# Delta attention, ELU network and top-2 experts on one core: narrower mask products, transpositions at the ends of periods, other gate chunks between the blocks

## Chip, core and metric

One core of one Trainium2 chip runs the whole program. The metric is its device time in microseconds, the median over runs.

## The reference, cut to what matters

```python
def _attn_ref(q, k, v, beta):                 # 4 x 8 heads, 768 positions, 48 wide
    k_n = k / (np.linalg.norm(k, axis=-1, keepdims=True) + 1e-06)
    state = zeros((B, H, D, D))
    for t in range(S):
        y[:, :, t] = q_t @ state
        v_old = k_t @ state
        state = state + beta_t * outer(k_t, v_t - v_old)

x = attention output as (3072, 384)
h = x @ w_in;  g = elu(h);  x = g @ w_out     # 384 -> 2048 -> 384
logits = x @ w_gate + log1p(exp(x @ w_noise)) * noise
the two best of 8 experts for each token:  relu(x @ w1[e]) @ w2[e], weighted and summed
```

The change touches the attention part and what is prepared beside it. Nothing in the ELU network or the experts is touched.

## The kernel before

The recurrence is done in chunks of 128 positions. A unit is one head of one chunk; 8 units (one batch entry, one chunk) are one n, and n runs from 0 to 23 (`NIT`). In each unit a 128 x 128 triangular system is solved in four steps of 32 rows (`BLK`), for which the four 32 x 32 diagonal blocks are inverted beforehand.

**Preparation.** TensorE computes the diagonal blocks in twelve groups, `diagonal_blocks(i)`, i from 0 to 11, called block 0 to block 11 here (64 matmuls each, which the profile shows as 128 with their weight loads). ScalarE copies each to SBUF (`take_blocks`). VectorE turns the blocks so that one lane holds one block (`to_set_lanes`), takes norms (`take_norms`) and runs the elimination column by column (`eliminate`, two operations a column, 31 columns). There are three groups of blocks. VectorE inverts the first one itself; it breaks off after `PREPARED` columns to turn and scale what the second group needs, and then ends its own 31 columns. GpSimd inverts groups 1 and 2: `POOL_COLUMNS` lists its columns, the first part (14 columns of group 1) after `scale_v(0)` and `scale_v(1)`, the others one part a period, each behind two `scale_v`, which wait for a chunk of v to be loaded. `place(g, s)` on VectorE turns a half of a finished group back; it waits for the last column of its group (`row_done`).

Between the blocks TensorE also does the gate: the product of w_out with the gate's weights, in 16 chunks. Chunk f is three transposes (`turn_output_weights`), a copy by ScalarE (`take_turned`) and three small matmuls (`gate_columns`), which come behind the transposes of chunk f + 1. `chunks_with(i)` says which chunks follow block i, on SyncE's queue, on TensorE and on ScalarE alike. When all 16 are turned, SyncE issues the loads of k for n = 0 to 3 and after them those of v for n = 2 and 3.

**Pairs.** After some filler matmuls (`keep_clock`), a loop over `PAIRS` = 12 periods m works on the two n = 2m and 2m + 1 (`solve`, `couple`, `outputs`, `updates`), and prepares the next two: `products_of_keys` on TensorE, `mask_products` on VectorE (which takes the products out of PSUM and zeroes what is not needed, writing `lq`; four pairs of operations in a period) and, from n = 4 on, `right_side`, which needs the v that GpSimd has scaled. The products have one PSUM buffer for each half, so the next products wait for the masks before. Each engine's order is written out by hand, in code order. A period is counted here from VectorE's first residual of it (`residuals(a, 1)`, L943).

From 275 us on the ELU network and the experts run.

Of the kernel before, what the change touches and what calls it, by code (L numbers as in the profile page):

```python
# [13 lines left out]
ALU = mybir.AluOpType  # L14
ACT = mybir.ActivationFunctionType
AX = mybir.AxisListType
P = 128
# [41 lines left out]
W_LOADED_WITH = {1: (2,), 2: (3,), 3: (4,), 4: (5,), 5: (0,), 6: (1,), 8: (6,), 9: (7, 8), 10: (9, 10, 11)}  # L59


PREPARED = 12
KEEP_BUSY = 29

# [3 lines left out]
def attention_outputs(nc, kv_dram, kqT_dram, beta_lanes, beta_turned, w_io, w_gn, masks, carried, inversion, w_parts,  # L70
# [13 lines left out]
    with ExitStack() as scope:  # L84
# [143 lines left out]

        def chunks_with(i):

            at = 2 * (i - KT_BUFS - 1)
            return (at, at + 1) if at >= 0 else ()

        def inverse_of(n, r):

# [23 lines left out]
        def _(sp):  # L259
# [81 lines left out]
            for i in range(KT_BUFS + 1, NIT // 2):  # L341
# [7 lines left out]
                    sp.dma_start(wgn, w_gn).then_inc(wgn_loaded, 16)  # L349
                for f in chunks_with(i):  # L350
                    load_output_weights(f)
            for f in chunks_with(NIT // 2):
                load_output_weights(f)
            sp.wait_ge(kqT_cleared, DEEP)
            for n in range(2, DEEP):
                load_kqT(n)
# [99 lines left out]
        def _(pe):  # L456
# [150 lines left out]
            for i in range(NIT // 2):  # L607
# [1 line left out]
                    products_of_keys(i // 2, i % 2)  # L609
                diagonal_blocks(i)  # L610
                gate_work(i)
            gate_work(NIT // 2)

            pe.wait_ge(blocks_taken, NIT // 2)
            gate_columns(FT1 - 1)
            pe.wait_ge(gate_taken, 1)
# [80 lines left out]
        def _(act):  # L697
# [78 lines left out]
            for i in range(NIT // 2):  # L776
# [4 lines left out]
                take_blocks(i)  # L781
                for f in chunks_with(i):
                    take_turned(f)
            for f in chunks_with(NIT // 2):
                take_turned(f)
            take_gate()
            act.wait_ge(cleared, len(by_pool))
            for n in range(2):
# [54 lines left out]
        def _(dve):  # L843
# [77 lines left out]
            def mask_products(n, c):  # L921
                dve.wait_ge(grams_done, 2 * n + c + 1)
                if n >= KEPT:

                    dve.wait_ge(y_done, n - KEPT + 1)
                for h in range(2):
                    to = lq[n % KEPT].rearrange("p (g a h) s t -> p g a h (s t)", g=2, h=2)[:, :, c * QP // 2:(c + 1) * QP // 2, h]
                    nc.vector.tensor_tensor(to, of_keys(h).rearrange("p g a s t -> p g a (s t)"),
                                            masks[:].rearrange("p g s t -> p g (s t)").unsqueeze(2).to_broadcast([P, 2, QP // 2, 2 * P]),
                                            ALU.mult).then_inc(masked, 1)  # L930

            def right_side(n):
                dve.wait_ge(ks_done[n % 2], (n - B) // 2 + 1)
# [51 lines left out]
            for m in range(PAIRS):  # L985
                a, b = 2 * m, 2 * m + 1
                past, more = m > 0, m < PAIRS - 1
                kept = past and b - 2 + B < NIT
                residuals(a, 1)
                if m == 1:  # L990
                    invert_root(2)
                if more:
                    mask_products(a + 2, 0)
                residuals(b, 1)
                if kept:
                    update_state(a - 2)
                if m == 1:
                    divide_by_root(2)
                if m == 3:
                    place(1, 0)  # L1000
                if m == 7:
                    place(2, 0)
                residuals(a, 2)
                if m == 1:
                    refine_root(2)
                if more:
                    mask_products(a + 2, 1)
                residuals(b, 2)
                if kept:
                    update_state(b - 2)  # L1010
                residuals(a, 3)
                if more and a + 2 >= B:
                    right_side(a + 2)
                if more:
                    mask_products(b + 2, 0)
                if more and b + 2 >= B:
                    right_side(b + 2)
                residuals(b, 3)
                if more:
                    mask_products(b + 2, 1)  # L1020
                if m == 0:
                    to_set_lanes(2, (5,))
                    square_norms(2)
                if m == 1:
                    gains(2)
                    turn_norms(2)
                if m == 4:
                    place(1, 1)
                if m == 7:
                    place(2, 1)  # L1030


TB = 384
# [955 lines left out]
```

## Time and profile before

| | |
|---|---|
| median of 3 runs | 1165.01 us (1163.78 to 1166.38) |
| the profiled execution | 1167.03 us |
| its span | 1165.3 us |
| preparation, until the first solve | 0 to 80 us |
| pairs | 80 to 275 us |
| ELU network and experts | 275 to 1165 us |
| TensorE busy over the span | 96% |
| TensorE clock granted, mean | 0.997 of full speed |

The span is the part of the execution that the profile records. Busy TensorE is not TensorE at its peak, since its matmuls are pipelined.

### The profile page before, as it was taken

What the parts mean: (1) busy time and instruction counts of PE and PEld (TensorE: products, weight loads), DVE (VectorE), ACT (ScalarE), POOL (GpSimd) and SP (SyncE); (2) the same over time, 40 slices, a digit from 0 to 9 for tenths busy, and PEclk for the clock granted to TensorE, in tenths of its full rate; (3) what the DMA queues carried; (4) which work ended last, traced back from release to release, by engine and by line L of the source; (5) the groups of instructions that cost most, each with busy time, mean ns of one, the idle gap of its engine ahead of it and who ended that gap; (6) DMA issues with size and microseconds to landing.
All of it is one profiled execution on the core that took longest, in us unless ns stands there. A gap on an engine that the chain in (4) does not pass through costs nothing.

```text
span 1165.3 us, 29047 instructions
## 1 busy us (share of the span) xinstructions
PE 1116.0 (96%) x11562; PEld 1069.2 (92%) x11562; DVE 647.7 (56%) x1552; ACT 462.6 (40%) x1048; POOL 355.7 (31%) x378
## 2 busy tenths in 40 slices
PE   4898999999999999999999999999999999999996
PEld 3786787888999999999999999999999999999995
DVE  4989787763465646565565657533434343434442
ACT  1236665884333343333333345323333333333331
POOL 5289995541002012020202102322223232322223
PEclk9999999999999999999999999999999999999998
DMA  7544657646996010010101011472424242434221
GB/s 158 126 128 105 166 135 172 164 139 237 366 360 208 25 58 35 27 41 20 41 20 42 22 43 66 172 235 73 170 79 166 86 157 94 147 103 140 61 69 53
DMA packets 82603, 137.30 MB, mean 118 GB/s; under 512 B 11050, under 2 KB 70034, under 8 KB 81466
## 3 DMA queue, kind: packets, MB, share of 16 engines
q1 hardware_dynamic: 68490, 87.97, 25.9%
q0 software_dynamic: 12992, 28.75, 7.7%
q10 hardware_dynamic: 1008, 18.97, 4.4%
q8 instruction: 83, 1.36, 0.5%
q14 instruction: 30, 0.25, 0.1%
HBM read 81.96 MB, written 53.77 MB: 116 GB/s over the span
## 4 chain that ended last, share of the span: by engine, by line
PE 74%; DVE 1%; issue 0%; ACT 0%; POOL 0%; ACTq 0%; POOLq 0%
PE ps_x L1426 18%; PE ps_x L1516 18%; PE ps_h L1415 18%; PE ps_h L1494 17%; PE ps_r L1474 2%; PE ps_r L1465 2%; DVE hg L1834 0%; ACT hg L1624 0%; POOL out_dram L1381 0%; DVE w_parts L1797 0%; PE ps_r L1533 0%; DVE x_raw L1827 0%; PE ps_r L1443 0%; ACT yT_d L1642 0%; PE ps_r L1441 0%
## 5 line engine op out<-in xcount | busy, mean ns | idle before, releaser
L1516 PE MATMUL ps_x<-hg,w_parts 128*128 128x400 f32 x1152 | 230.2, 346 | 0.0
L1426 PE MATMUL ps_x<-w_parts,hg 128*128 128x400 f32 x1152 | 229.7, 345 | 0.0
L1415 PE MATMUL ps_h<-xg,w_parts 128*128 128x384 f32 x1152 | 222.4, 338 | 0.0
L1494 PE MATMUL ps_h<-xg,w_parts 128*128 128x400 f32 x1116 | 220.6, 345 | 1.1 <-DVE w_parts L1797 1.1
L1426 PEld LDWEIGHTS ps_x<-w_parts,hg 128*128 128x128 f32 x1152 | 209.7, 188 | 0.0
L1834 DVE SCALAR_TENSOR_TENSOR hg<-ps_h,hg 128x400 fp32r<-128x400 f32 x128 | 73.6, 575 | 243.1 <-ACT hg L1624 242.6
L1415 PEld LDWEIGHTS ps_h<-xg,w_parts 128*128 128x128 f32 x1152 | 204.0, 188 | 2.5 <-DVE elu_parts L1691 2.5
L1494 PEld LDWEIGHTS ps_h<-xg,w_parts 128*128 128x128 f32 x1116 | 202.7, 188 | 4.0 <-issue 3.1
L1516 PEld LDWEIGHTS ps_x<-hg,w_parts 128*128 128x128 f32 x1152 | 206.1, 188 | 0.0
L1361 POOL DMA_INDIRECT xs_scratch<-x,rows_now x48 | 49.5, 1032 | 393.4 <-DVE rows_now L1771 294.7
L1624 ACT ACTIVATE hg<-ps_h 128x400 fp32r<-128x400 f32 x128 | 64.6, 505 | 256.5 <-PE ps_h L1494 256.5
L1573 ACT ACTIVATE hg<-elu_parts 128x384 fp32r<-128x384 f32 x128 | 67.2, 525 | 183.6 <-DVE elu_parts L1691 183.6
L1694 DVE TENSOR_TENSOR hg<-elu_parts,hg 128x384 fp32r<-128x384 f32 x128 | 71.6, 559 | 80.8 <-ACT hg L1573 80.8
L1381 POOL DMA_INDIRECT out_dram<-x_raw,token_now x48 | 48.6, 1012 | 175.7 <-DVE x_raw L1827 137.0
L1688 DVE TENSOR_SCALAR elu_parts<-expo 128x384 f32<-128x384 f32 x128 | 46.9, 366 | 85.0 <-ACT expo L1566 82.2
L1566 ACT ACTIVATE expo<-ps_h 128x384 f32<-128x384 f32 x128 | 62.1, 485 | 79.2 <-PE ps_h L1415 78.8
L1371 POOL DMA_INDIRECT x<-out_dram,token_now x45 | 47.4, 1052 | 127.0 <-DVE token_now L1816 115.9
L722 ACT ACTIVATE x_of<-psum 32x192 f32<-32x192 f32 x192 | 61.7, 321 | 59.8 <-PE psum L563 55.4
L1691 DVE SCALAR_TENSOR_TENSOR elu_parts<-ps_h,elu_parts 128x384 f32<-128x384 f32 x128 | 71.4, 558 | 4.4
L943 DVE TENSOR_TENSOR rhs<-rhs,psum 32x192 f32<-32x192 f32 x144 | 50.6, 351 | 31.7 <-PE psum L575 27.7
L253 POOL TENSOR_TENSOR inversion<-inversion 128x62 f32<-128x62 f32 (+15 forms) x62 | 55.5, 896 | 4.9
L526 PE MATMUL psum<-kqT 48*64 48x256 f32 (+1 forms) x768 | 45.3, 352 | 11.5 <-DMA kqT<-in_kqT_dram 7.4
(175 smaller groups left out, 1309.8 us busy)
## 6 DMA issues: line engine op xcount, KB each, us to landing
xs_scratch<-pads SPq DMA_DIRECT2D x2, 5502.0 KB, 41.9
x_rows<-xs_scratch SPq DMA_DIRECT2D x17, 614.1 KB
kqT<-in_kqT_dram SPq DMA_DIRECT2D x48, 192.0 KB, 4.0
carried<-in_w_dram ACTq DMA_DIRECT2D x3, 3072.0 KB, 11.2
w_raw<-in_w_dram ACTq DMA_DIRECT2D x3, 3072.0 KB, 11.4
xs_scratch<-pads SPq DMA_DIRECT2D x6, 1375.5 KB, 16.5
out_dram<-pads SPq DMA_DIRECT2D x1, 4800.0 KB, 30.1
xs_scratch<-pads SPq DMA_DIRECT2D x6, 786.0 KB, 9.0
```

Source lines behind the costliest of these rows:

```text
L253: vec.tensor_tensor(t, t, outer, ALU.subtract).then_inc(row_done[g], 1)
L722: nc.scalar.activation(x[n % KEPT][rows, half(g), :], ps_p[n % 2][rows, g * HALF_U * DH:(g + 1) * HALF_U * DH].rearrange("p (u d) -> p u d ...
L1415: mm = nc.tensor.matmul(ps_h[f % 2][:, 0:TB], wi[:, 1 - a, k, f * P:(f + 1) * P], xr[:, b, k, :], start=(i == 0), stop=(i == len(passes) - 1))
L1426: mm = nc.tensor.matmul(ps_x[t][:, 0:DG], act_r[:, f % RING, a, t * P:(t + 1) * P], wo[:, b, f, :], start=(f == 0 and i == 0), stop=(f == ...
L1494: mm = nc.tensor.matmul(ps_h[f % 2][:, 0:TR], w1, xg[:, b, k, :], start=(m == 0), stop=(m == len(passes) - 1))
L1516: mm = nc.tensor.matmul(ps_y[k][:, 0:TR], w2r[i][:, a, s, k * P:(k + 1) * P], hg[:, s % RING, b, :], start=(s == 0 and m == 0), stop=(s == ...
L1566: nc.scalar.activation(expo[:, f % 2], ps_h[f % 2][:, 0:TB], ACT.Exp).then_inc(exp_done, 1)
L1573: nc.scalar.activation(act_r[:, f % RING, 0], act_raw[:, f % 2], ACT.Copy).then_inc(act_hi, 1)
L1624: nc.scalar.activation(hg[:, f % RING, 0], ps_h[f % 2][:, 0:TR], ACT.Relu).then_inc(relu_hi, 1)
L1691: nc.vector.scalar_tensor_tensor(act_raw[:, f % 2], ps_h[f % 2][:, 0:TB], 0.0, expm[:, f % 2], ALU.max, ALU.add).then_inc(act_done, 1)
L1694: nc.vector.tensor_tensor(act_r[:, f % RING, 1], act_raw[:, f % 2], act_r[:, f % RING, 0], ALU.subtract).then_inc(act_split, 1)
L1834: nc.vector.scalar_tensor_tensor(hg[:, f % RING, 1], ps_h[f % 2][:, 0:TR], 0.0, hg[:, f % RING, 0], ALU.max, ALU.subtract).then_inc(relu_s ...
```

## The change

Five edits, and nothing else:

```diff
-PREPARED = 12
+PREPARED = 10
+GATE_WITH = {5: (0,), 6: (1,), 7: (2,), 8: (3, 4, 5), 9: (6, 7, 8), 10: (9, 10, 11), 11: (12, 13, 14, 15)}
...
         def chunks_with(i):
-            at = 2 * (i - KT_BUFS - 1)
-            return (at, at + 1) if at >= 0 else ()
+            return GATE_WITH.get(i, ())
...
-                    nc.vector.tensor_tensor(to, of_keys(h).rearrange("p g a s t -> p g a (s t)"),
-                                            masks[:].rearrange("p g s t -> p g (s t)").unsqueeze(2).to_broadcast([P, 2, QP // 2, 2 * P]),
-                                            ALU.mult).then_inc(masked, 1)
+                    nc.vector.tensor_tensor(to[..., BLK:], of_keys(h).rearrange("p g a s t -> p g a (s t)")[..., BLK:],
+                                            masks[:].rearrange("p g s t -> p g (s t)")[:, :, BLK:].unsqueeze(2)
+                                            .to_broadcast([P, 2, QP // 2, 2 * P - BLK]), ALU.mult).then_inc(masked, 1)
...
-                if m == 3:
-                    place(1, 0)
-                if m == 7:
-                    place(2, 0)
                 residuals(a, 2)
...
-                if m == 4:
-                    place(1, 1)
-                if m == 7:
-                    place(2, 1)
+                if m in (2, 4):
+                    place(1, m // 2 - 1)
+                if m in (6, 7):
+                    place(2, m - 6)
```

The three places that did the chunks of `chunks_with(NIT // 2)` after block 11 fall away, since the table puts the last chunks with block 11. The first 32 of the 256 columns of a mask product, which the change no longer writes, are read by no matmul (`couple` reads rows 32 to 127 of the first half).

TensorE in the preparation, from block 5's end on, before. L475 is a block, L489 the transposes of a chunk (k_in0 to k_in3 are the four buffers of w_out's chunks), L495 its gate columns; the row ahead is blocks 3 to 5.

```order
L475 MATMUL psum<-inversion 32x32 x192
L489 MATMUL psum<-inversion,k_in0 128x128 x3
L489 MATMUL psum<-inversion,k_in1 128x128 x3
L495 MATMUL psum<-inversion 128x16 x3
L475 MATMUL psum<-inversion 32x32 x64
L489 MATMUL psum<-inversion,k_in2 128x128 x3
L495 MATMUL psum<-inversion 128x16 x3
L489 MATMUL psum<-inversion,k_in3 128x128 x3
L495 MATMUL psum<-inversion 128x16 x3
L475 MATMUL psum<-inversion 32x32 x64
```

And with the change (L473 is a block, L487 transposes, L493 gate columns):

```order
L473 MATMUL psum<-inversion 32x32 x192
L487 MATMUL psum<-inversion,k_in0 128x128 x3
L473 MATMUL psum<-inversion 32x32 x64
L487 MATMUL psum<-inversion,k_in1 128x128 x3
L493 MATMUL psum<-inversion 128x16 x3
L473 MATMUL psum<-inversion 32x32 x64
L487 MATMUL psum<-inversion,k_in2 128x128 x3
L493 MATMUL psum<-inversion 128x16 x3
L473 MATMUL psum<-inversion 32x32 x64
L487 MATMUL psum<-inversion,k_in3 128x128 x3
L493 MATMUL psum<-inversion 128x16 x3
L487 MATMUL psum<-inversion,k_in0 128x128 x3
```

One chunk instead of two now follows each of the blocks 5, 6 and 7, and three follow block 8.

VectorE from the second last mask products of period 6 on, before: L943 is a residual, L928 masks, L954 the state's update, L918 `place`. The row with L918 is `place(2, 0)`, in the middle of period 7.

```order
L936 TENSOR_TENSOR rhs3<-rhs3,psum 128x384
L943 TENSOR_TENSOR rhs1<-rhs1,psum 32x192 x2
L928 TENSOR_TENSOR lq1<-psum,masks 128x2x256 x2
L943 TENSOR_TENSOR rhs2<-rhs2,psum 32x192 x2
L928 TENSOR_TENSOR carried<-psum,masks 128x2x256 x2
L943 TENSOR_TENSOR rhs3<-rhs3,psum 32x192 x2
L954 TENSOR_TENSOR state0<-state0,psum 48x4x48 x2
L918 STREAM_TRANSPOSE carried<-inversion 128x32x32
L943 TENSOR_TENSOR rhs2<-rhs2,psum 32x192 x2
L928 TENSOR_TENSOR carried<-psum,masks 128x2x256 x2
L943 TENSOR_TENSOR rhs3<-rhs3,psum 32x192 x2
```

With the change (L937 residuals, L922 masks, L912 `place`):

```order
L930 TENSOR_TENSOR rhs3<-rhs3,psum 128x384
L937 TENSOR_TENSOR rhs1<-rhs1,psum 32x192 x2
L922 TENSOR_TENSOR lq1<-psum,masks 128x2x224 x2
L912 STREAM_TRANSPOSE carried<-inversion 128x32x32
L937 TENSOR_TENSOR rhs2<-rhs2,psum 32x192 x2
L922 TENSOR_TENSOR carried<-psum,masks 128x2x224 x2
L937 TENSOR_TENSOR rhs3<-rhs3,psum 32x192 x2
L948 TENSOR_TENSOR state0<-state0,psum 48x4x48 x2
```

`place(2, 0)` now stands behind period 6's last masks and ahead of period 7's first residual. `place(1, 0)` moves in the same way from the middle of period 3 to the end of period 2; `place(1, 1)` and `place(2, 1)` stay at the ends of periods 4 and 7.

## Rows read from the trace of the kernel before

**Rows 1.** Busy time by stretch (us, instructions, TensorE clock, DMA share, GB/s).
```profile
80.00:275.00 195.00, 178.05 (x4765) 147.57 (x4764) 145.09 (x307) 127.71 (x322) 135.54 (x135) 1.00 0.55 139
275.00:1165.30 890.30, 877.91 (x5044) 867.74 (x5044) 441.18 (x1138) 313.89 (x683) 178.55 (x186) 1.00 0.33 111
```

**Rows 2.** The page's DMA queues: the one that carries instructions.
```profile
q8 instruction: 83, 1.36, 0.5%
```

**Rows 3.** Timeline, TensorE, 25 to 59 us: start, duration, operation [idle before].
```profile
25.65 0.45 PE L475 MATMUL psum<-inversion 48*32 48x32 f32 x27 [0.78 <-ACT inversion L706]
28.13 1.30 PE L475 MATMUL psum<-inversion 48*32 48x32 f32 x101 [2.04 <-issue]
...
32.14 1.30 PE L475 MATMUL psum<-inversion 48*32 48x32 f32 x102 [1.49 <-issue]
...
44.20 0.33 PE L475 MATMUL psum<-inversion 48*32 48x32 f32 x7 [0.43 <-issue]
...
50.32 0.45 PE L475 MATMUL psum<-inversion 48*32 48x32 f32 x27 [0.83 <-issue]
...
56.59 0.90 PE L489 MATMUL psum<-inversion,k_in 128*128 128x128 f32 x3
...
58.43 0.88 PE L489 MATMUL psum<-inversion,k_in 128*128 128x128 f32 x3
```

**Rows 4.** Timeline, TensorE, end of the preparation.
```profile
73.17 2.58 PE L495 MATMUL psum<-inversion 128*128 128x16 f32 x12
76.23 3.90 PE L481 MATMUL psum<-masks 128*128 128x192 f32 x10 [0.47 <-ACT x_raw L755]
```

**Rows 5.** Timeline, SyncE's DMA queue: the third and fourth block of v.
```profile
81.89 0.33 SPq L277 DMA_DIRECT2D v_in<-in_kv_dram  x1
```

**Rows 6.** Timeline, GpSimd, from its first wait to its last column.
```profile
85.05 0.83 POOL L418 TENSOR_TENSOR rhs<-v_in,x_raw 128x384 f32<-128x384 f32 x1 [2.84 <-DMA v_in<-in_kv_dram]
...
122.92 0.32 POOL L253 TENSOR_TENSOR inversion<-inversion 128x62 f32<-128x62 f32 x1
...
168.54 1.62 POOL L418 TENSOR_TENSOR rhs<-v_in,x_raw 128x384 f32<-128x384 f32 x2
...
191.53 0.32 POOL L253 TENSOR_TENSOR inversion<-inversion 128x62 f32<-128x62 f32 x1
```

**Rows 7.** Timeline, VectorE, periods 2 to 11.
```profile
123.77 1.29 DVE L928 TENSOR_TENSOR lq<-psum,masks 128x512 f32<-128x512 f32 x2
...
169.66 0.56 DVE L936 TENSOR_TENSOR rhs<-rhs,psum 128x384 f32<-128x384 f32 x1
...
185.46 0.56 DVE L936 TENSOR_TENSOR rhs<-rhs,psum 128x384 f32<-128x384 f32 x1 [0.65 <-POOL rhs L418]
...
188.48 1.29 DVE L928 TENSOR_TENSOR lq<-psum,masks 128x512 f32<-128x512 f32 x2
191.64 0.74 DVE L943 TENSOR_TENSOR rhs<-rhs,psum 32x192 f32<-32x192 f32 x2 [1.87 <-PE psum L575]
...
195.84 1.95 DVE L918 STREAM_TRANSPOSE carried<-inversion 128x1024 f32<-128x1024 f32 x1
...
208.17 0.74 DVE L943 TENSOR_TENSOR rhs<-rhs,psum 32x192 f32<-32x192 f32 x2
...
240.00 0.74 DVE L943 TENSOR_TENSOR rhs<-rhs,psum 32x192 f32<-32x192 f32 x2 [1.87 <-PE psum L575]
...
255.19 1.51 DVE L943 TENSOR_TENSOR rhs<-rhs,psum 32x192 f32<-32x192 f32 x4 [1.87 <-PE psum L575]
```

**Rows 8.** Timeline, TensorE, period 7: the wait behind the transposition.
```profile
198.60 0.53 PE L563 MATMUL psum<-rhs,inv_bd 128*32 128x48 f32 x16 [1.07 <-DVE rhs L943]
```

**Rows 9.** Timeline, TensorE, period 10: the wait for a mask.
```profile
250.91 0.88 PE L526 MATMUL psum<-kqT 48*64 48x256 f32 x16 [0.34 <-DVE lq L928]
```

**Rows 10.** Timeline, VectorE, columns of the inversion, by size.
```profile
57.57 0.70 DVE L253 TENSOR_TENSOR psum<-psum,inversion 128x512 f32<-128x512 f32 x1
...
66.00 0.62 DVE L253 TENSOR_TENSOR psum<-psum,inversion 128x440 f32<-128x440 f32 x1
```

More of the change, by code:

```diff
@@ L351, in _ @@
                     load_output_weights(f)
-            for f in chunks_with(NIT // 2):
-                load_output_weights(f)
             sp.wait_ge(kqT_cleared, DEEP)
@@ L611, in _ @@
                 gate_work(i)
-            gate_work(NIT // 2)
             pe.wait_ge(blocks_taken, NIT // 2)
@@ L783, in _ @@
                     take_turned(f)
-            for f in chunks_with(NIT // 2):
-                take_turned(f)
             take_gate()
```

## The prediction

> **What bounds the kernel now.** I read the busy times by stretch first [rows 1]. From 275 us on the work is not touched and TensorE is busy nearly all of its 890 us, so the change can only move the point at which this stretch starts. In the 195 us of the pairs TensorE is busy for 178 us, yet no engine is full, and the order of waits decides. So I followed the timelines of the engines, preparation first.
>
> In the preparation two chains run side by side: VectorE's inversion of group 0, and TensorE's blocks and chunks. TensorE's ends last: its last gate columns end at 73.17 + 2.58 = 75.75 us, the filler matmuls start at 76.23, and take 3.90 [rows 4]. TensorE's side sets one more thing. The loads of v for n = 2 and 3 come behind four loads of k on SyncE's queue, and all of these behind the last transposed chunk; the first is issued at 81.89 [rows 5]. GpSimd, done with its first 14 columns, waits 2.84 us for that v, from 82.2 until 85.05 [rows 6].
>
> From there GpSimd has a chain of its own: columns and `scale_v` without a gap that I could find in its timeline, until group 1's last column ends at 123.24 and group 2's at 191.85 [rows 6]. In period 5 its `scale_v(12)` is done at about 169.36 (half of the two from 168.54), and VectorE's `right_side(12)` starts at 169.66; in period 6 VectorE waits 0.65 us for it before `right_side(14)` [rows 6, 7]. So towards the middle of the pairs GpSimd, which looks idle in the average, is just about to bind. After 191.85 it is free, and the last periods go by TensorE: 255.19 - 240.00 = 15.19 us [rows 7].
>
> **Gate chunks.** TensorE's blocks are short of something that no engine releases. In blocks 4 and 5, which have no chunks between them, the run of 128 matmuls is split after 27, with 2.04 and 1.49 us of "issue" before the rest [rows 3]. 128 matmuls with 128 weight loads are 256 instructions, and the queue that carries instructions moved 1.36 MB in 83 transfers, 16.4 KB each [rows 2]: I read the split as the edge of one transfer, and the wait as the next one that isn't there yet. The resumes are 28.13 and 32.14, so 4.0 us from edge to edge without other work. Later edges with a wait fall at 44.20 (7 matmuls ahead of block 7's end) and at 50.32: 6.12 us between them, with waits of 0.43 and 0.83 [rows 3].
>
> The Trainium skill (Runtime: NRT & Kernel Launch, Instruction fetch mechanics) has the same size, 16 KiB blocks of 256 instructions, fetched on a queue of their own while the engine runs, and calls the cost of an edge mostly hidden. The trace agrees on the size and not on the cost, at 2.04 us of wait. By that rule the chunks' place would cost nothing, which is the second rival below.
>
> With the change blocks 6, 7 and 8 have one chunk between them. A chunk is 9 matmuls in the trace (3 and 6) and takes 58.43 - 56.59 = 1.84 us, a block some 1.6 (1.30 for 101 matmuls) [rows 3]. With two chunks a block that is 5.3 us of work from edge to edge, which covers 4.0 but not 6.1; with one it is 3.4, and TensorE runs into the edge each time. From the edge at 32.14, the rest of block 5 (101), chunks 0 to 2 (21 with the columns that are done by then) and blocks 6 to 8 (384) are 506 matmuls; the fourth edge after it, 512 matmuls on, lies just behind block 8. At 4.0 us an edge it is passed at 32.14 + 16.0 = 48.15 us. What remains then is more than remained before at 56.59, the end of block 9 [rows 3]: from there to 75.75 it took 19.16 us [rows 4]. To add are chunks 3 to 7 (5 x 1.84 = 9.2) and block 9 (1.6), 30.0 in all, in which three chunks a block (7 us) cover every edge. The end is 78.1, so some 2.3 us later than 75.75. I take **+2.0**, because two loads of w_out fewer are on the queues just before 25 us. Bounds: 0 if the edges are hidden after all; 2.3 + 2.1 = +4.4 if one of the four edges costs 6.12 instead of 4.0. The same 2.0 us go to the filler matmuls and the first solve, and, through the loads of k and v, to GpSimd's restart: 85.05 becomes about 87.0, and its last columns end at 125.2 and 193.85.
>
> **PREPARED = 10.** Two columns of VectorE (four operations of 0.62 to 0.70 us [rows 10], some 2.7 us) move behind the preparation of group 1. GpSimd's 14 columns start and end 2.7 us earlier, at 79.5, and then wait for the same v: its idle time grows from 2.84 to some 7.6 us. Worth 0. VectorE's own total stays. If the block it needs were late it would wait there, but block 7 ends earlier now, with two chunks fewer ahead of it.
>
> **Masks.** A pair of mask operations takes 1.29 us for 512 elements each [rows 7]. Columns of the elimination take 0.70 us at 512 and 0.62 at 440 [rows 10], so 448 elements save 0.07 us each, 0.13 a pair. On the path are two of the four pairs of a period: TensorE waits 0.34 us for the third [rows 9], behind the second in VectorE's order. Gain 0.27 a period, bounded by 0 and by that 0.34. In periods 0 and 1, where VectorE is nearly full, up to 0.5.
>
> **Transpositions.** In the middle of period 7 `place(2, 0)` takes 1.95 us on VectorE and makes TensorE wait 1.07 us [rows 7, 8]; that period lasts 208.17 - 191.64 = 16.53 us [rows 7], against 15.19. At the end of a period VectorE has 1.87 us to spare [rows 7], so there a transposition costs 0.1. Period 3 gains about 1.3 in the same way: period 2's last masks end at 125.06 before [rows 7], group 1's last column at 123.24, and both move by 2.0, the masks less some 1.2.
>
> For `place(2, 0)` this does not hold. Period 6's masks end at 188.48 + 1.29 = 189.77 [rows 7], and group 2 ends at 191.85 even now. The transposition has to wait, and behind it in VectorE's order stands period 7's first residual, for which TensorE waits.
>
> **The sum.** Up to period 6 the gains (masks some 2.5, `place(1, 0)` 1.3) are taken by GpSimd: `right_side(12)` waits about 3 us in period 5, `right_side(14)` about 1 in period 6. Then group 2 ends at 191.85 + 2.0, `place(2, 0)` runs until 195.8, and the residual starts at about 195.9 instead of 191.64: 2.26 + 2.0 later. Period 7 then lasts 15.19 + 0.05 - 0.27 = 14.97 instead of 16.53, so -1.56. Periods 9 and 10 give 0.27 each, -0.54; I leave out period 8: with period 9 it takes 240.00 - 208.17 = 31.83 us, 1.45 more than twice 15.19 with no transposition in it [rows 7], and what lengthens it may well take a gain of 0.27 too. So 2.0 + 2.26 - 1.56 - 0.54 = **+2.2 us**. Against the span that gives 1167.5, and against the profiled execution 1169.2, which lies 2.0 above the median of the runs; on the median, 1165.0 + 2.2 = **1167.2 us**.
>
> **The rivals.** What counts as no change is within 0.2%, 2.3 us, about what a measurement of this kernel can tell; 1162.7 to 1167.3.
> - Code arrives late once between blocks 5 and 9: +4.4 in the preparation, +4.6 at the end, 1169.6 us. For it speaks the 6.12; against it, that SyncE then has few loads to issue.
> - The edges are hidden by other work, as by the skill's rule: the gate ends at 75.75 as before, and 0 + 2.26 - 1.56 - 0.54 = +0.2, 1165.2. Against it stand the 2.04 and 1.49.
> - The other side: GpSimd's chain doesn't bind, because it restarts earlier. Then masks (3.1) and both transpositions (2.6) come out, against the later start of 2.0: 3.7 us faster, 1161.3. It decides when v for n = 2 lands before about 82.5 instead of 85.05, which needs a gate that ends 2.5 us earlier. GpSimd would be ready, since PREPARED frees it at 79.5; what could shorten the gate are waits as the 0.43 and 0.83 us at its edges, and these are less than 2.5.
> - Half of it: period 7 gains, and the wait for group 2 is shorter than 2.26 because GpSimd's operations shift; about 0, 1165.
>
> **How the numbers follow.** The forecast as worked out has 0.45, and its own range is +1 to +3.5, so about half of it on each side of 2.3. Late code 0.15, hidden edges 0.18, the fast case 0.13, about nothing 0.09. Faster: 0.13. Slower: 0.22 + 0.15 = 0.37. Same: 0.50. The range leaves out half of the fast case and the far end of the late code: 1163.0 to 1171.0.
>
> **What the changed profile would show.** Splits in each of the blocks 6, 7 and behind 8, with "issue" waits of 0.7 to 2 us, and 16 us from 32.1 to the last. The last gate columns at 77 to 79 us. GpSimd idle for 7 us or more before the first `scale_v` of the pairs. Masks at 0.62 us each. VectorE's `right_side` in periods 5 and 6 waiting for GpSimd's scaled v by 3 and 1 us, and the transposition at the end of period 6 waiting some 2.3 us for GpSimd's last column. Periods 9 and 10 at 14.9 us. I am wrong if GpSimd has a gap between 87 and 190 us, if the gate ends at 76 or earlier, or if the transposition finds its group ready.

## The result

| | before | changed |
|---|---|---|
| median of 17 runs each | 1165.14 us (1162.97 to 1168.25) | 1168.03 us (1165.85 to 1170.41) |
| the profiled execution | 1167.03 us | 1168.43 us |
| its span | 1165.3 us | 1166.7 us |
| last gate columns end | 75.75 us | 78.85 us |
| group 2's last column ends | 191.85 us | 194.40 us |
| last period's first residual | 255.19 us | 256.54 us |

The ratio is 1.0026, with a 95% interval of 1.0018 to 1.0034: the change costs 2.9 us. The forecast was 1167.2, +2.2 us.

The two profiles differ by 1.40 us and the medians by 2.9. They agree all the same: the profiled execution of before lies 1.9 us above its median and the changed one 0.4. In the pairs, until the last period's first residual, TensorE stops three times for "issue" before (1.18, 0.39 and 1.18 us, at 127.60, 218.75 and 224.49) and three times after (0.16, 0.44, 0.47, at 137.27, 161.24 and 226.17): 2.75 against 1.07 us. After it the changed kernel stops once more, for 0.31 us at 259.14. "issue" is what the profile writes when it shows nothing that the engine waited for. These stops are of the same kind as the waits in the blocks, and their lengths scatter from execution to execution.

**TensorE among the blocks.** The timeline of the changed kernel from block 4 on, which answers to [rows 3] (start, duration, operation, count [idle before]; L473 is a block, L487 the transposes of a chunk):

```profile
26.93 1.36 PE L473 MATMUL psum<-inversion 48*32 48x32 f32 x101 [1.23 <-issue]
...
31.22 1.30 PE L473 MATMUL psum<-inversion 48*32 48x32 f32 x102 [1.71 <-issue]
...
33.31 0.43 PE L473 MATMUL psum<-inversion 48*32 48x32 f32 x22
35.76 1.36 PE L473 MATMUL psum<-inversion 48*32 48x32 f32 x106 [2.02 <-issue]
...
42.50 0.31 PE L473 MATMUL psum<-inversion 48*32 48x32 f32 x2
44.48 1.53 PE L473 MATMUL psum<-inversion 48*32 48x32 f32 x126 [1.67 <-issue]
45.94 0.47 PE L487 MATMUL psum<-inversion,k_in 128*128 128x128 f32 x1
48.04 0.59 PE L487 MATMUL psum<-inversion,k_in 128*128 128x128 f32 x2 [1.62 <-issue]
...
53.28 1.29 PE L473 MATMUL psum<-inversion 48*32 48x32 f32 x101
55.68 0.45 PE L473 MATMUL psum<-inversion 48*32 48x32 f32 x27 [1.11 <-issue]
```

The splits lie 127 or 128 matmul records apart, or a multiple of it. From the edge at 31.22, 102 records of block 5, three transposes and 22 of block 6 are 127; the next edge is at 35.76. From 44.48, 126 of block 8 and one transpose are 127; the next is at 48.04. Between 35.76 and 44.48 are two times 127, so one edge lies inside block 7, and there the profile shows no wait. Behind the single chunks the waits at the other three are 2.02, 1.67 and 1.62 us, where before the edges in blocks 7 and 8 cost 0.43 and 0.83. The four edges take 48.04 - 31.22 = 16.82 us. Then comes one that I had taken as covered: three chunks lie between 48.04 and block 9's edge, and TensorE still waits 1.11 us, until 7.64 us after the last.

**The end of the preparation.** The last gate columns and the filler matmuls on TensorE, as [rows 4]:

```profile
76.27 2.58 PE L493 MATMUL psum<-inversion 128*128 128x16 f32 x12
79.32 3.99 PE L479 MATMUL psum<-masks 128*128 128x192 f32 x10 [0.47 <-ACT x_raw L751]
```

SyncE's queue, the first load of v for n = 2, as [rows 5]:

```profile
84.49 0.33 SPq L277 DMA_DIRECT2D v_in<-in_kv_dram  x1
```

**GpSimd**, from its wait to its last column, as [rows 6] (L416 is `scale_v`, L253 a column):

```profile
87.68 0.83 POOL L416 TENSOR_TENSOR rhs<-v_in,x_raw 128x384 f32<-128x384 f32 x1 [8.60 <-DMA v_in<-in_kv_dram]
...
125.48 0.32 POOL L253 TENSOR_TENSOR inversion<-inversion 128x62 f32<-128x62 f32 x1
...
171.08 1.62 POOL L416 TENSOR_TENSOR rhs<-v_in,x_raw 128x384 f32<-128x384 f32 x2
...
187.08 1.61 POOL L416 TENSOR_TENSOR rhs<-v_in,x_raw 128x384 f32<-128x384 f32 x2
...
194.08 0.32 POOL L253 TENSOR_TENSOR inversion<-inversion 128x62 f32<-128x62 f32 x1
```

Its idle time is 8.60 us, and from the restart at 87.68 to the end of group 2 at 194.40 pass 106.72 us; before, from 85.05 to 191.85, 106.80. It runs the same chain 2.6 us later. In both kernels the chain has one gap, ahead of its second `scale_v`, which waits for the v of n = 3: 0.97 us, and 1.06 before.

**VectorE**, as [rows 7] (L912 is `place`, L930 `right_side`, L922 masks, L937 residuals):

```profile
127.09 1.99 DVE L912 STREAM_TRANSPOSE inversion<-inversion 128x1024 f32<-128x1024 f32 x1
...
172.01 0.55 DVE L930 TENSOR_TENSOR rhs<-rhs,psum 128x384 f32<-128x384 f32 x1 [2.64 <-POOL rhs L416]
...
188.01 0.55 DVE L930 TENSOR_TENSOR rhs<-rhs,psum 128x384 f32<-128x384 f32 x1 [1.00 <-POOL rhs L416]
...
190.89 1.16 DVE L922 TENSOR_TENSOR lq<-psum,masks 128x448 f32<-128x448 f32 x2
194.44 1.95 DVE L912 STREAM_TRANSPOSE carried<-inversion 128x1024 f32<-128x1024 f32 x1 [2.39 <-POOL inversion L253]
196.42 0.74 DVE L937 TENSOR_TENSOR rhs<-rhs,psum 32x192 f32<-32x192 f32 x2
197.19 1.16 DVE L922 TENSOR_TENSOR carried<-psum,masks 128x448 f32<-128x448 f32 x2
...
210.71 0.74 DVE L937 TENSOR_TENSOR rhs<-rhs,psum 32x192 f32<-32x192 f32 x2
...
226.47 0.74 DVE L937 TENSOR_TENSOR rhs<-rhs,psum 32x192 f32<-32x192 f32 x2 [2.74 <-PE psum L573]
...
241.51 0.74 DVE L937 TENSOR_TENSOR rhs<-rhs,psum 32x192 f32<-32x192 f32 x2 [2.01 <-PE psum L573]
...
256.54 1.51 DVE L937 TENSOR_TENSOR rhs<-rhs,psum 32x192 f32<-32x192 f32 x4 [2.01 <-PE psum L573]
```

`place(1, 0)` finds its group ready. The two `right_side` wait 2.64 and 1.00 us for GpSimd, and `place(2, 0)` 2.39 us for the last column. The residual behind it starts at 196.42 instead of 191.64, and period 7 lasts 14.29 us. Periods 9 and 10 last 15.04 and 15.03.

**The third pair of masks**, TensorE's wait for it in period 10, as [rows 9]:

```profile
252.26 0.88 PE L524 MATMUL psum<-kqT 48*64 48x256 f32 x16 [0.25 <-DVE lq L922]
```

### The profile page after: what moved, and what is told of

The parts are those of the page before. It is cut to its first block, busy times and chain, and to the rows that moved or that the text cites. A ratio compares the mean times of both kernels' runs of the same rounds, so it can differ in the third digit from the quotient of the medians.

```text
span 1166.7 us, 29047 instructions
## 1 busy us (share of the span) xinstructions
PE 1115.1 (96%) x11562; PEld 1068.1 (92%) x11562; DVE 642.0 (55%) x1552; ACT 462.8 (40%) x1048; POOL 355.8 (30%) x378
## 3 DMA queue, kind: packets, MB, share of 16 engines
q8 instruction: 83, 1.36, 0.5%
## 4 chain that ended last, share of the span: by engine, by line
PE 74%; DVE 1%; issue 0%; ACT 0%; POOL 0%; ACTq 0%; POOLq 0%
PE ps_x L1416 18%; PE ps_x L1506 18%; PE ps_h L1405 17%; PE ps_h L1484 17%; PE ps_r L1464 2%; PE ps_r L1455 2%; DVE hg L1824 0%; ACT hg L1614 0%; POOL out_dram L1371 0%; DVE w_parts L1787 0%; PE ps_r L1523 0%; DVE x_raw L1817 0%; PE ps_r L1433 0%; ACT yT_d L1632 0%; PE ps_r L1431 0%
## 5 line engine op out<-in xcount | busy, mean ns | idle before, releaser
L937 DVE TENSOR_TENSOR rhs<-rhs,psum 32x192 f32<-32x192 f32 x144 | 50.6, 352 | 32.6 <-PE psum L573 28.5
L253 POOL TENSOR_TENSOR inversion<-inversion 128x62 f32<-128x62 f32 (+15 forms) x62 | 55.5, 895 | 4.9
```

The source lines that it names most:

```text
L253: vec.tensor_tensor(t, t, outer, ALU.subtract).then_inc(row_done[g], 1)
```

## The experiments

The kernel before ran beside all of them: 1166.82, 1166.57 and 1166.06 us in the three sets. The ratios are to it, over all runs; they differ from the quotients of the medians by up to 0.0008. "Gate end" is the end of the last gate columns in the one profiled execution.

| kernel | median us | ratio | 95% interval | gate end |
|---|---|---|---|---|
| before + table alone (a1) | 1169.33 | 1.0023 | 1.0011 to 1.0034 | 80.33 |
| changed, table undone (a2) | 1166.19 | 1.0003 | 0.9992 to 1.0015 | 75.10 |
| changed, v early (a3) | 1165.22 | 0.9993 | 0.9983 to 1.0002 | 78.28 |
| changed, `place(2, 0)` back (a4) | 1168.94 | 1.0018 | 1.0008 to 1.0029 | 78.04 |
| before + places (b2) | 1165.80 | 0.9992 | 0.9982 to 1.0002 | 74.70 |
| before + masks (b1) | 1165.16 | 0.9990 | 0.9979 to 1.0001 | 75.70 |
| before + v early (d1) | 1164.17 | 0.9986 | 0.9974 to 0.9998 | 75.06 |
| changed, table undone, v early (b3) | 1162.29 | 0.9957 | 0.9941 to 0.9973 | 75.90 |
| the same, GpSimd's columns spread (c1) | 1160.29 | 0.9948 | 0.9928 to 0.9968 | 74.12 |
| c1 with the new table (d2) | 1163.16 | 0.9978 | 0.9967 to 0.9989 | 78.30 |
| c1 with few chunks later (d3) | 1164.93 | 0.9996 | 0.9985 to 1.0007 | 80.83 |

**1. The table alone, and all but the table.** My theory was that the table is the whole loss, and the rival that the moved transposition is.

```diff
 # the kernel before, with the table alone
+GATE_WITH = {5: (0,), 6: (1,), 7: (2,), 8: (3, 4, 5), 9: (6, 7, 8), 10: (9, 10, 11), 11: (12, 13, 14, 15)}
```

> The kernel before with the new table of gate chunks and nothing else. Code-fetch theory: the last gate columns end some 3 us later than before (78.9 instead of 75.75, as in the changed kernel), GpSimd restarts at 87.7 instead of 85.05, and the whole is 2.6 to 3.1 us slower than before (1167.7 to 1168.3), no transposition waiting for GpSimd. Rival, it is the transposition that stands too early: the table alone costs nothing or under 1 us.

```diff
 # the changed kernel, with the old distribution
+GATE_WITH = {5: (0, 1), 6: (2, 3), 7: (4, 5), 8: (6, 7), 9: (8, 9), 10: (10, 11), 11: (12, 13, 14, 15)}
```

> The changed kernel with the old distribution of the chunks (two behind each block from block 5 on); PREPARED, masks and transpositions as changed. Code-fetch theory: gate columns end at 75.3 to 75.8 us, GpSimd restarts at about 85.0, the transposition at the end of period 6 still waits about 2.4 us for GpSimd's last column, and the whole is 0 to 1.2 us faster than before (1164 to 1165), that is 2.6 to 3 us faster than the changed kernel. Rival, the early transposition alone is what costs: then this is still some 2 us slower than before (1167).

The table alone costs 0.23%, and the changed kernel without it is at 1.0003. By the medians that is 2.5 us slower, where I expected 2.6 to 3.1, and 0.6 us faster, inside my 0 to 1.2. In the one profile of the table alone the gate ends at 80.33 us and GpSimd restarts at 89.29, some 1.5 us later than I expected of each. The changed kernel over that one is 1.0026 / 1.0003 = 1.0023, the same 0.23% again. With the old table GpSimd restarts at 84.19 us and ends group 2 at 190.65; VectorE waits for it at the same three places, 3.02, 0.97 and 2.39 us. The rival, that the moved transposition costs it all, has the table alone cost nothing or under 1 us, and is out. So the loss is the table's, and what the other edits save is given back in waits for GpSimd.

**2. GpSimd's chain taken off the path.** The loads of v for n = 2 and 3 no longer stand behind the last chunk of w_out.

```diff
+            for n in (2, 3):
+                load_v(n)
             sp.wait_ge(wo_turned_ps, FT1)
             for n in range(K_DEEP):
                 load_k(n)
-            for n in (2, 3):
-                load_v(n)
```

> The changed kernel with SyncE's loads of v for n = 2 and 3 put ahead of the wait for the last transposed chunk (and so ahead of the loads of k). Theory that GpSimd's chain, started by that v, takes the gains of masks and transpositions: GpSimd goes on at about 79.5 us without a wait instead of 87.7, ends group 2 at about 186 instead of 194.4, right_side waits for it nowhere, the transposition at the end of period 6 doesn't wait, and the whole is 3.5 to 5.5 us faster than the changed kernel, so 1 to 2.5 us faster than before (1162.5 to 1164) although the gate still ends at 78.9. Rival, GpSimd only happens to be as late as TensorE: within 1 us of the changed kernel.

GpSimd's timeline in this kernel:

```profile
78.74 1.62 POOL L416 TENSOR_TENSOR rhs<-v_in,x_raw 128x384 f32<-128x384 f32 x2 [0.47 <-DMA v_in<-in_kv_dram]
...
114.09 0.83 POOL L416 TENSOR_TENSOR rhs<-v_in,x_raw 128x384 f32<-128x384 f32 x1 [1.73 <-issue]
...
131.03 0.83 POOL L416 TENSOR_TENSOR rhs<-v_in,x_raw 128x384 f32<-128x384 f32 x1 [5.30 <-issue]
...
191.37 0.32 POOL L253 TENSOR_TENSOR inversion<-inversion 128x62 f32<-128x62 f32 x1
```

The restart comes 8.9 us earlier, the end only 2.7: I expected 186. The chain now stops in two places, 1.73 and 5.30 us, ahead of `scale_v`. By the code `scale_v(n)` waits there until TensorE has solved n - 4, which used the same one of the four `rhs` buffers; GpSimd has run as far ahead as its buffers let it. It ends at 191.69, and VectorE still waits 1.88 us for it before `right_side(12)` and 1.73 us before the transposition, where I expected no wait at all. Against the changed kernel the gain by the two ratios is 1.0026 / 0.9993 = 1.0033, or 3.8 us, inside my 3.5 to 5.5. Against the kernel before it is 0.8 us by the ratio and 1.6 by the medians, where I expected 1 to 2.5, and the interval doesn't tell it from zero. I hadn't looked at how far ahead GpSimd may run.

**3. `place(2, 0)` back in the middle of period 7**, with all other edits.

> The changed kernel with the first transposition of group 2 back in the middle of period 7; that of group 1 stays at the end of period 2. My theory: the wait of 2.39 us for GpSimd's last column goes, and period 7 starts near 194 instead of 196.4, but it gets the 1.07 us wait of TensorE back and loses what TensorE had done ahead, so period 7 lasts 16.3 instead of 14.3 us: in sum 0 to 0.6 us faster than the changed kernel. Rival, the wait is a full loss: 1.3 to 2.4 us faster than the changed kernel.

VectorE's timeline in this kernel, period 7's first residual and the transposition:

```profile
193.51 0.74 DVE L937 TENSOR_TENSOR rhs<-rhs,psum 32x192 f32<-32x192 f32 x2 [2.01 <-PE psum L573]
...
197.57 1.95 DVE L912 STREAM_TRANSPOSE carried<-inversion 128x1024 f32<-128x1024 f32 x1
```

The period starts at 193.51 and the next at 209.67, so it lasts 16.16 us with the transposition inside. The last period starts at 255.21 us, 1.33 before the changed kernel's; 0.8 of that was there at the gate end. In the medians nothing is seen (1.0018 against 1.0026, the intervals overlap), which agrees with my 0 to 0.6 us but also with a gain of 1 us or more. Where it stands makes no difference that these runs can tell: ahead of the period it waits, inside it it makes the others wait.

**4. The places alone and the masks alone**, each on the kernel before.

> The kernel before with the moved transpositions alone. My theory: group 1's gives about 1.3 us in period 3, which GpSimd takes back by period 6; the one of group 2 waits about 2.1 us for GpSimd's last column at the end of period 6 and period 7 is some 2.2 us shorter: within 1 us of before (ratio 0.9995 to 1.0007). Rivals: the early transposition of group 2 costs its full wait, 2 us slower (1.0018); or both moves pay, 2.5 us faster (0.998).

> The kernel before with the narrower masks alone. Theory: masks are worth 0.15 us a period (idle of VectorE before a residual 2.01 us instead of 1.87 in the changed kernel), and periods 2 to 6 are held by GpSimd; with periods 0, 1 and 7 to 11 some 1 us is left: -0.5 to -1.5 us, ratio 0.9987 to 0.9996. My prediction's price (0.27 a period, all twelve on the path) would give -3.1 us. Rival: 0, since VectorE is not full anywhere.

Places alone: 0.9992, just outside my 0.9995. VectorE waits 2.63 us for GpSimd before `right_side(12)` and 1.52 us before the transposition: group 2 ends at 190.71, where it was 191.85, and that is no more than the gate's earlier end (74.70 against 75.75). Masks alone: 0.9990; neither is told from zero by its interval. VectorE's timeline in the kernel with the masks alone shows why they give so little:

```profile
128.41 0.74 DVE L943 TENSOR_TENSOR rhs<-rhs,psum 32x192 f32<-32x192 f32 x2 [3.85 <-PE psum L575]
...
169.39 0.55 DVE L936 TENSOR_TENSOR rhs<-rhs,psum 128x384 f32<-128x384 f32 x1 [0.56 <-POOL rhs L418]
...
185.35 0.55 DVE L936 TENSOR_TENSOR rhs<-rhs,psum 128x384 f32<-128x384 f32 x1 [0.97 <-POOL rhs L418]
...
191.40 0.74 DVE L943 TENSOR_TENSOR rhs<-rhs,psum 32x192 f32<-32x192 f32 x2 [2.00 <-PE psum L575]
...
240.34 0.74 DVE L943 TENSOR_TENSOR rhs<-rhs,psum 32x192 f32<-32x192 f32 x2 [2.60 <-PE psum L575]
...
255.37 1.51 DVE L943 TENSOR_TENSOR rhs<-rhs,psum 32x192 f32<-32x192 f32 x4 [2.00 <-PE psum L575]
```

From period 3's residual to period 7's it takes 191.40 - 128.41 = 62.99 us. Before, the same stretch took 191.64 - 128.49 = 63.15, so four periods gave 0.16 us together, and two waits for GpSimd, 0.56 and 0.97 us, stand in it. Period 10, where GpSimd is done, lasts 15.03 us against 15.19 [rows 7].

**5. v early alone, v early with the changed kernel's other edits, and GpSimd's columns spread.**

> The kernel before with one edit: the loads of v for n = 2 and 3 are issued ahead of SyncE's wait for the last transposed chunk. Theory: in the kernel before GpSimd only just reaches VectorE, with one wait of 0.65 us in period 6 and none that delays a residual, so a chain that runs ahead of need gives little: between 0 and -1 us, ratio 0.999 to 1.0. Rival: part of the seemingly idle 16.53 us of period 7 is GpSimd's doing, and the edit alone gives -2 us or more.

> The changed kernel with the old distribution of the chunks and the loads of v for n = 2 and 3 ahead of the wait for the last transposed chunk. From the two runs that did one of these each: 2.6 us for the chunks and 3.5 us for the v are to add up, so 5 to 6 us below the changed kernel and 3 to 4 us below before (ratio 0.9965 to 0.9975). GpSimd goes on at about 79 and is stopped later, about 125 to 131 us less 3, by the v buffer of four n before; the transposition of group 2 still waits 1.5 to 2 us. If GpSimd's end did not set the time, the two would not add: ratio 0.9985 or more.

```diff
 # c1: the kernel of b3, and
-POOL_COLUMNS = ((1, 0, 14),), ((1, 14, 21),), ((1, 21, 28),), ((1, 28, 31), (2, 0, 3)), ((2, 3, 12),), ((2, 12, 19),), ((2, 19, 26),), ((2, 26, 31),)
+POOL_COLUMNS = ((1, 0, 17),), ((1, 17, 23),), ((1, 23, 29),), ((1, 29, 31), (2, 0, 6)), ((2, 6, 12),), ((2, 12, 18),), ((2, 18, 24),), ((2, 24, 31),)
```

> As the run with old chunks and early v, and GpSimd's parts of columns made even: 17, 6, 6, 2 + 6, 6, 6, 6, 7 instead of 14, 7, 7, 3 + 3, 9, 7, 7, 5, so that the time GpSimd gained at the start is spent on columns instead of on waiting for a free buffer. Theory: right_side and both transpositions wait for GpSimd nowhere, every period from 3 on goes by TensorE at about 15.0 us, and the whole is 4.5 to 6 us below before (ratio 0.995 to 0.996). Rival, TensorE's own chain is the bound already: no faster than the same kernel with the old parts.

This is the experiment that shows what the edits are worth. The changed kernel without the table gives 1.0003 while v is late. v early alone gives 0.9986. All together give 0.9957, so masks, places and PREPARED = 10 are worth 0.9957 / 0.9986 = 0.9971, some 3.4 us (2.4 by the medians), once GpSimd's chain starts early. The two ran in different sets, and by their intervals it is anything from 1 to 5.7 us. No run takes PREPARED = 10 alone. In the kernel of b3 GpSimd's first `scale_v` of the pairs starts at 80.41, in that of d1 at 81.67, but its group 2 ends at 190.12 and not at 187.65, so nothing of that start is left at the end of its chain. And GpSimd is not out of the way yet. VectorE's timeline in b3, its waits for GpSimd and period 6's first residual:

```profile
167.75 0.56 DVE L930 TENSOR_TENSOR rhs<-rhs,psum 128x384 f32<-128x384 f32 x1 [2.19 <-POOL rhs L416]
...
176.65 0.74 DVE L937 TENSOR_TENSOR rhs<-rhs,psum 32x192 f32<-32x192 f32 x2 [4.34 <-PE psum L573]
...
190.15 1.99 DVE L912 STREAM_TRANSPOSE carried<-inversion 128x1024 f32<-128x1024 f32 x1 [0.21 <-POOL inversion L253]
```

The 4.34 us ahead of the residual, where other periods have 2.00, are TensorE at half its clock (see the last section). With the columns spread evenly the kernel comes to 1160.29 us, 6.3 below the one before in the same set; the changed one, in another set, had 1168.03. VectorE's timeline there, the transposition:

```profile
185.39 1.96 DVE L912 STREAM_TRANSPOSE carried<-inversion 128x1024 f32<-128x1024 f32 x1
```

Group 2 ends at 184.75, and the transposition waits for nothing. That spreading the columns is by itself worth something (0.9948 against 0.9957) is within the intervals and not shown. For v early alone the interval reaches from my range (0.999 to 1.0) to the rival's -2 us, so how much GpSimd held the kernel before is left open between 0.2 and 3 us.

**6. The code edges themselves.** Eight more small matmuls in block 0 shift every later matmul record on TensorE by 16. They write again what the block has written. This kernel ran once, so only its trace is used, not its time.

```diff
+                for _ in range(8 if i == 0 else 0):
+                    mm = nc.tensor.matmul(ps_d[rows_of(to), h, ca * BLK:(ca + 1) * BLK], k_u, k_u, start=True, stop=True)
                 mm.then_inc(chunk_done, 1)
```

> The kernel before with the last matmul of block 0 done 8 times more (the same result written again): 16 matmul records and 16 weight loads, 32 instructions ahead of all that follows. Theory of a code transfer each 256 instructions: the splits of blocks 3, 4 and 5, which came after 27 matmuls, come after 11, with the same waits of 1.5 to 3 us, and those of blocks 7, 8 and 9 (121, 101, 82) after 105, 85 and 66. Rival, the wait is for data of the block or for ScalarE: the splits stay at 27.

TensorE's timeline in this kernel, splits in blocks 4, 6, 7 and 8:

```profile
27.96 1.45 PE L475 MATMUL psum<-inversion 48*32 48x32 f32 x117 [2.27 <-issue]
...
39.44 0.32 PE L475 MATMUL psum<-inversion 48*32 48x32 f32 x4 [1.08 <-issue]
...
45.29 0.44 PE L475 MATMUL psum<-inversion 48*32 48x32 f32 x23 [0.50 <-issue]
...
51.17 0.71 PE L475 MATMUL psum<-inversion 48*32 48x32 f32 x43 [0.65 <-issue]
```

The split in block 4 now leaves 117 matmuls behind it, where it was 101 [rows 3]; in blocks 7 and 8 it leaves 23 and 43 of 128, so 105 and 85 lie ahead of it, where it was 121 and 101. The waits sit at places counted in instructions, not at a point of the algorithm or of the time.

**7. The table with GpSimd off the path, and the few chunks put later.**

> The fastest kernel so far (v early, GpSimd's columns spread evenly, the old two chunks a block) with the new chunk table. Here GpSimd restarts independently of the gate and nothing in the pairs waits for it. Theory: the table costs what it costs TensorE before the first solve, 2.5 to 3.3 us, so 1162.8 to 1163.6 against 1160.3. Rival: the table hurts only through the late restart of GpSimd; then it costs under 0.5 us here.

```diff
 # d3: the fastest kernel, and
+GATE_WITH = {5: (0, 1), 6: (2, 3), 7: (4, 5), 8: (6,), 9: (7,), 10: (8,), 11: (9, 10, 11, 12, 13, 14, 15)}
```

> The same fastest kernel with one chunk instead of two behind blocks 8, 9 and 10 (two behind 5, 6, 7 as in the kernel before; seven behind block 11). Theory: what costs is a stretch of 256 instructions whose work is shorter than the code transfer, wherever it lies. Splits with a wait of 0.5 to 1.5 us move into blocks 9, 10 and 11, the gate ends 1 to 3 us later than with two a block, and so does the kernel. Rival: only blocks 5 to 8 are short of code, because SyncE loads k there; then this table costs nothing and the new table's price is one of place.

The new table costs 1163.16 - 1160.29 = 2.9 us where VectorE waits for GpSimd nowhere (0.9978 / 0.9948 = 1.0030; the two ran in different sets, and the two intervals together allow 0.8 to 6.2 us, which still leaves out the rival's 0.5). So its price is paid at TensorE's start of the pairs; that it also delays GpSimd is a second way to the same 3 us, not a further price.

With few chunks later TensorE's timeline shows the splits in blocks 8 to 11:

```profile
52.42 0.46 PE L473 MATMUL psum<-inversion 48*32 48x32 f32 x27 [3.30 <-issue]
...
56.99 0.67 PE L473 MATMUL psum<-inversion 48*32 48x32 f32 x37 [1.09 <-issue]
...
61.96 0.74 PE L473 MATMUL psum<-inversion 48*32 48x32 f32 x47 [1.36 <-issue]
...
78.25 2.58 PE L493 MATMUL psum<-inversion 128*128 128x16 f32 x12
```

Splits with waits of 1.09, 1.36 and 0.36 us stand in blocks 9, 10 and 11, where there was one of 0.38 us in c1. So it isn't the place. The gate end is 6.7 us later than c1's, though, and I expected 1 to 3. The part behind the split in block 8, where the two tables first differ, is as expected: from 52.42 to 80.83 are 28.41 us, in c1 from 48.70 to 74.12 25.42, so 3.0 more. The other 3.7 us are there when block 8's split ends, most of them in its wait of 3.30 us (0.56 in c1), and the order on TensorE does not explain them. What goes with them is other traffic: over the 8.59 us from the edge in block 7 to that in block 8 the core's DMA engines were busy for 1.08 of the time (as the profile has it), over c1's 5.85 us for 0.72. One profile can't say whether that is scatter. The kernel is 4.6 us slower than c1 by the medians and 5.6 by the ratios, which doesn't settle it.

## Why the prediction came out as it did

**The sign, the mechanism and most of the sizes were right; one term was too small.** That the total came so near is in part luck, since misses of both signs cancel in it (the sum below). By my steps:

- *Gate chunks, +2.0.* The mechanism held (experiments 1, 6 and 7). The size is +3.1 in the two profiles, and over all profiled executions the gate ends at 75.19 us on average with the old table (seven) and at 78.76 with the new one (five): **+3.6**. (Experiment 6, with its added matmuls, and d3, with a third table, are left out.) Much of the scatter lies ahead of the first chunk. Counted from the edge in block 5, it takes 43.45 to 44.17 us to the gate end with the old table and 46.79 to 48.39 with the new one, 43.7 and 47.5 on average: +3.8, and no value of one group lies among those of the other. My own working had 78.15 - 32.14 = 46.0 there. Two steps fell short, and one was wrong without harm. "At 4.0 us an edge": the four edges took 16.82 us, 4.2 each, though they ended at 48.04, where I had 48.15, since the first one came earlier. "Three chunks a block (7 us) cover every edge": block 9's came 7.64 us after the one before and cost 1.11 us. So from 48.04 to the gate end it took 30.81 us and not 30.0. "TensorE runs into the edge each time" did not hold for the edge in block 7, which shows a wait of 0.16 us in two of the five kernels with this table and none in the others. I also took 2.0 where my own working gave 2.3, for two loads fewer on the queues. There is something in that: from the split in block 3 to that in block 5 it takes 7.92 to 8.87 us with the new table and 8.33 to 9.68 with the old one, 8.3 and 8.9 on average. Behind it the table costs 3.8, where my working had 2.3 to 2.4.
- *GpSimd's chain.* Restart 87.68 against 87.0, idle 8.60 against 7.6, end of group 2 at 194.40 against 193.85: right, with the gate's error in it. That the chain has no gap was a slip, by the 1.06 us ahead of its second `scale_v`; it costs the sum nothing, as both kernels have it.
- *PREPARED, 0.* GpSimd's first part ended earlier and it waited longer, as foreseen: 87.68 - 8.60 = 79.08 against 85.05 - 2.84 = 82.21.
- *Waits that replace the gains.* Forecast 3, 1 and 2.3 us; measured 2.64, 1.00 and 2.39.
- *Masks, -0.27 a period.* It is -0.15: periods of 15.04 and 15.03 us instead of 15.19, and 15.03 with the masks alone. Only the pair whose end TensorE waits for counts. It waited 0.34 us for it [rows 9] and still waits 0.25, while VectorE's slack before the residual grew from 1.87 to 2.01 us: the other pair's gain went there.
- *Period 7, 14.97.* It took 14.29. The late residual let TensorE get ahead: the masks behind it start at once, at 197.19, where before they waited 0.60 us for their products, so 0.57 of the late start is caught up.
- *Period 8, left out.* It lasted 226.47 - 210.71 = 15.76 instead of 16.64. What lengthened it before were TensorE's waits for "issue", 0.39 us at 218.75 and 1.18 at 224.49, against 0.47 in the changed kernel, and not a matter of the period's work.

The sum against the profiles: the residual of period 7 is 4.78 us later (forecast 4.26), period 7 is 2.24 shorter (1.56), period 8 is 0.88 shorter (0), periods 9 and 10 are 0.31 shorter (0.54); +1.35 at the last period (forecast 2.16), and 1.40 at the end. So the late residual was forecast 0.5 too small and periods 9 and 10 0.2 too fast, while period 7 gave 0.7 and period 8 0.9 more than forecast; period 8's part is the chance of two executions. The profile of before has 1.7 us more of such waits in the pairs until then, and 1.4 more in all; with them the difference would be 2.8 to 3.1, which is where the medians' 2.9 lies.

The rival "the edges are hidden" fell with the first experiment. By the rule of the Trainium skill that it went by (Runtime: NRT & Kernel Launch, Instruction fetch mechanics), the edges are mostly hidden; the runs show waits of 0 to 1.7 us, once 3.3, where two or three chunks lie ahead of the edge, so there it holds in part, and of 0.9 to 4.0 in blocks 3 to 5, which have nothing between them, where it doesn't. "Late code once", at +4.4 in the preparation, was nearer than I gave it: one edge more than planned was late, at 1.11 us instead of 2.1. The rival with GpSimd off the path needed v before 82.5 us; moving the loads made that so by other means. The rival's 1161.3 has the new table in it: the kernels with it gave 1165.2 (a3) and 1163.2 (d2, with GpSimd's columns spread), those with the old one 1162.3 and 1160.3.

## What to carry to other kernels

Small matmuls can use up instructions faster than they arrive: where runs of short instructions are split by waits that no engine releases, look at the instruction count between the splits and at the other DMA traffic there, and spread the longer work between them. Before pricing savings on two engines, follow the third one that looks idle, from what starts it to where it is waited for; here its chain of 106.7 us took all of them, and moving two loads made them count. When a chain is started earlier, ask how far its buffers let it run.

## What was not expected of the hardware

- The time from edge to edge of TensorE's code is no constant. With short work between them it was 3.56 to 4.54 us (35.76 - 31.22 and 48.04 - 44.48); with more work between them it was 6.1 us before and 7.64 in the changed kernel, and TensorE still waited at its end. Over all kernels even two neighbouring edges in bare blocks (those in blocks 3, 4 and 5) lie 3.47 (28.18 to 31.65 in d3) to 6.50 us apart (21.68 to 28.18, in the same profile), so the 4.0 of the prediction was one sample of a wide spread. The time goes with how busy the core's DMA engines are from one edge to the other. Of the 28 such distances in 14 profiles, the nine with a DMA share up to 0.05 are 3.47 to 4.03 us, the nine with 0.51 to 0.69 are 3.48 to 4.71, and the ten with 0.83 to 1.03 are 4.56 to 6.50. Other transfers would then hold up those of the code. No run changes the traffic alone, and the 7.64 us, at a share of 0.53, don't fit the row.
- Such waits also fall into the pairs, up to 1.70 us: 2.75 us in all in the profile of before, 1.07 in the changed one's, 3.49 in that of the kernel with the masks alone (all until the last period). What scatters is whether and how long TensorE waits, not where it can. The stop at 224.49 of before comes behind the same matmul as those at 226.17 of the changed kernel and at 223.42 of the masks alone, and 218.75 and 224.49 lie 126 matmul records apart. From 127.60 to 224.49 there are 2512, which is 20 times 125.6, a little under 127 since, as I read it, more of the 256 instructions are of kinds that the profile doesn't count. In experiment 6, where all is shifted by 16 records, the stops are at other matmuls. These waits are probably a part of the scatter between runs; no run measures how much.
- TensorE's clock fell to the lower of its two levels for some us in the pairs of 5 of the 14 profiled executions (looked at from 84 to 262 us), each time behind a stop of TensorE. In the kernel with v early alone it stopped 1.44 us for "issue". TensorE's timeline, and its busy time by stretch (us, busy with count, granted clock, DMA share, GB/s):

```profile
173.75 0.44 PE L575 MATMUL psum<-x_of,carried 128*32 128x48 f32 x10 [1.44 <-issue]
```

```profile
170.00:174.00 4.00, 2.56 (x56) 1.00 0.91 256
174.00:176.00 2.00, 2.00 (x50) 0.78 0.57 148
176.00:178.00 2.00, 2.00 (x40) 0.50 0.35 104
178.00:180.00 2.00, 2.00 (x48) 0.86 0.98 202
```

  The clock was 1.00 ahead of it and 0.50, the lower of the two levels, from 176 to 178 us; that period lasted 191.02 - 174.23 = 16.79 us, where before it was 191.64 - 175.83 = 15.81.

  The other four are a4, behind a stop of 1.70 us at 129.66, and a3, b2 and b3 in period 5, where TensorE had stood 2.10, 2.99 and 2.35 us behind VectorE's wait for GpSimd. In b3 the clock was 0.50 from 170 to 176 us, and from VectorE's last residual of period 5 to the first of period 6 it took 176.65 - 169.86 = 6.79 us; in a2, with 3.24 us of standing still and a clock of 1.00, the same took 174.32 - 170.39 = 3.93. So 2.9 us were lost to the clock, more than the wait itself. A wait for GpSimd can cost that way too. What decides it is open: the clock stayed at 1.00 behind 3.24 us in a2, 2.86 in the changed kernel and 1.57 in c1.
